# Window attention and two feed-forward layers: the order of GpSimd's early work, and who rounds the second layer's weights

## What is computed

```python
w = np.exp(weight_gen - np.max(weight_gen, axis=-1, keepdims=True))
w = w / (np.sum(w, axis=-1, keepdims=True) + 1e-09)
x_pad = np.concatenate([np.zeros((B, pad, D)), x], axis=1)      # pad = 6
out = np.einsum('bshk,bskhg->bshg', w, x_unf)                   # x_unf: windows of 7 tokens
...
h = x @ moe_w_in;   g = h * np.cos(h);            x = g @ moe_w_out
h = x @ moe2_w_in;  g = np.maximum(0.01 * h, h);  y = g @ moe2_w_out
```

## Time and profile before

| | us |
|---|---|
| median of 3 runs | 1169.44 (1168.51 to 1169.97) |
| the profiled execution | 1169.68 |
| its span, first to last instruction | 1167.8 |
| TensorE busy | 1144.5 (98%) |
| VectorE busy | 898.7 (77%) |
| ScalarE busy | 735.3 (63%) |
| GpSimd busy | 88.1 (8%) |

### The profile page before, as it was taken

One profiled execution on the slowest core, in us unless ns is written; L12 is line 12 of the kernel. 1 busy time (PEld: TensorE's weight loads), 2 busy tenths in 40 slices (PEclk: granted clock), 3 DMA queues, 4 the chain that ended last, 5 costly groups with the idle time before them and its releaser, 6 DMA issues.

```text
span 1167.8 us, 23296 instructions
## 1 busy us (share of the span) xinstructions
PE 1144.5 (98%) x10170; PEld 953.3 (82%) x10170; DVE 898.7 (77%) x860; ACT 735.3 (63%) x804; POOL 88.1 (8%) x89
## 2 busy tenths in 40 slices
PE   7789999999999999999999999999999999999998
PEld 5668888888888888888888888888888888888876
DVE  7778797778978788697786968868697786968433
ACT  5566675666757666575665757566575665757544
POOL 5761000000000000000000000000000000000000
PEclk9989999999999999999999999999999999999999
DMA  9700101001010010101001010010101001000000
GB/s 270 200 2 1 35 1 49 1 1 49 1 49 1 4 45 1 49 1 49 1 1 49 1 49 1 15 35 1 48 2 49 1 1 48 1 15 1 15 1 28
DMA packets 17389, 34.25 MB, mean 29 GB/s; under 512 B 5132, under 2 KB 11658, under 8 KB 17032
## 3 DMA queue, kind: packets, MB, share of 16 engines
q1 hardware_dynamic: 15114, 30.90, 8.4%
q0 software_dynamic: 2080, 1.57, 0.7%
q10 hardware_dynamic: 94, 0.29, 0.1%
HBM read 26.46 MB, written 6.29 MB: 28 GB/s over the span
## 4 chain that ended last, share of the span: by engine, by line
PE 92%; DVE 3%; POOL 2%; ACT 1%; issue 1%; DMA 0%; ACTq 0%; POOLq 0%
PE slot L1052 42%; PE acc_a L1052 28%; PE acc_b L1052 18%; DVE prods L304 1%; DVE g_lo L813 1%; POOL out_hi_lo L542 1%; DVE prods L298 1%; POOL prods L298 1%; POOL prods L304 1%; DMA taps_w<-in_weight_gen 0%; PE slot L997 0%; PE slot L984 0%; POOL in_a_lo L536 0%; DVE gate L885 0%; PE acc_b L1025 0%
## 5 line engine op out<-in xcount | busy, mean ns | idle before, releaser
L1052 PE MATMUL acc_a<-g_hi,out_hi_lo 64*128 64x512 f32 x2000 | 695.9, 388 | 0.0
L1052 PEld LDWEIGHTS acc_a<-g_hi,out_hi_lo 64*128 64x128 f32 x2000 | 368.0, 184 | 35.9
L1052 PE MATMUL acc_b<-g_hi,out_hi_lo 64*128 64x512 f32 x1000 | 387.9, 388 | 0.3 <-DVE g_lo L813 0.3
L1052 PE MATMUL acc_a<-g_lo,out_hi_lo 64*128 64x512 f32 x1000 | 386.5, 387 | 0.0
L1052 PE MATMUL acc_b<-g_lo,out_hi_lo 64*128 64x512 f32 x1000 | 386.4, 386 | 0.0
L813 DVE TENSOR_TENSOR g_lo<-gate,g_hi 128x1024 fp32r<-128x1024 f32 x240 | 293.0, 1221 | 117.2 <-ACT g_hi L624 116.8
L624 ACT ACTIVATE g_hi<-gate 128x1024 fp32r<-128x1024 f32 x240 | 254.4, 1060 | 90.8 <-PE acc_b L1052 77.5
L1052 PE MATMUL slot<-x_a_hi,in_a_lo 64*128 64x512 f32 x1024 | 299.9, 394 | 5.6 <-DVE g_lo L813 3.8
L1052 PE MATMUL slot<-x_b,in_b_hi 64*128 64x512 f32 x1024 | 296.2, 387 | 0.2 <-DVE x_b L827 0.2
L1052 PE MATMUL slot<-x_a_lo,in_a_hi 64*128 64x512 f32 x1024 | 296.2, 387 | 0.0
L1052 PE MATMUL slot<-x_a_hi,in_a_hi 64*128 64x512 f32 x1024 | 296.1, 387 | 0.0
(11 more groups left out here) (99 smaller groups left out, 1095.6 us busy)
## 6 DMA issues: line engine op xcount, KB each, us to landing
x_win<-in_x SPq DMA_DIRECT2D x14, 960.0 KB, 4.7
out<-result SPq DMA_DIRECT2D x16, 384.0 KB, 2.3
out_raw<-in_moe_w_out SPq DMA_DIRECT2D x3, 512.0 KB, 10.4
out_hi_lo<-in_moe_w_out POOLq DMA_DIRECT2D x2, 768.0 KB, 16.3
taps_w<-in_weight_gen SPq DMA_DIRECT2D x2, 560.0 KB, 7.9
in_a_raw<-in_moe_w_in SPq DMA_DIRECT2D x1, 1024.0 KB, 12.2
in_b_raw<-in_moe_w_in SPq DMA_DIRECT2D x2, 512.0 KB, 15.1
out_raw<-in_moe_w_out SPq DMA_DIRECT2D x1, 1024.0 KB, 21.9
```

The source lines that it names most:

```text
L1052: return nc.tensor.matmul(to, w[rows, :], x[rows, :], start=start, stop=stop)
```

## The change

1. `stays` holds for iteration 0 alone; first-layer units of iteration 1 write their results to `gate`.
2. GpSimd no longer waits for the second softmax's subtraction ahead of its column lows. Piece 2 of W1.out's lows goes behind the sum of pairs of chunk 1, piece 3 behind all of chunk 1's attention, with a wait for its end (`att` 22).
3. W2's high parts come by four transfers that round on the way, on GpSimd's queue behind piece 3. GpSimd's copies and casts for W2 go, the differences stay. SP loads `in_b_lo_raw` of W2 in its final layout, and waits for W1.out's second rounding transfer ahead of W2's raw loads. The zero borders of W2's `in_b_hi` are made by subtracting the identity from itself instead of by memsets.
4. The whole first halo is issued on SP. In chunk 0 the second and third product are split: the part that needs own tokens alone comes first, then the rest behind the halo's wait.

```diff
@@ stays @@
-        return i <= 1 and q < len(FIRST_UNITS)
+        return i == 0 and q < len(FIRST_UNITS)
@@ attention @@
+            def product(k, to, j, until):
+
+                w = taps_w[:, (c * J + j) * heads:(c * J + until) * heads, k]
+                return engine.tensor_tensor(
+                    prods[:, to, j * dim:until * dim].rearrange("p (r g) -> p r g", g=group),
+                    view[:, (k + j) * heads:(k + until) * heads, :],
+                    w.unsqueeze(2).to_broadcast([P, (until - j) * heads, group]), ALU.mult)
...
-                tap(4, 2)
+                product(4, 2, 0, J if c else 2).then_inc(att, 1)
 
             def start():
                 wait_for_chunk()
 
                 tap(6, 0)
+                if c == 0:
+                    product(5, 1, 1, J)
+                    product(4, 2, 2, J)
 
             def rest_of_window():
                 wait_for_halo()
-                tap(5, 1)
+                product(5, 1, 0, J if c else 1).then_inc(att, 1)
@@ SP @@
             load_own(0)
+            load_halo(sp, 0, 0)
             load_halo(sp, 0, P // batch)
...
+            sp.wait_ge(out_hi_loaded[1], 16)
             sp.dma_start(W2.in_a_raw[:, :], w_in2[0:DA, :]).then_inc(w2_loaded[0], 16)
-            sp.dma_start(W2.in_b_raw[0:DB, P:], w_in2[DA:dim, :])\
-                .then_inc(w2_loaded[1], 16)
-            sp.dma_start(W2.in_b_raw[DB:P, 0:hidden], w_in2[DA:dim, :])\
-                .then_inc(w2_loaded[1], 16)
+            for t in range(PAIR):
+                sp.dma_start(W2.in_b_lo_raw[t * DB:(t + 1) * DB, :].rearrange("p (u c) -> p u c", c=P),
+                             w_in2[DA:dim, :].rearrange("p (u t c) -> p u t c", t=PAIR, c=P)[:, :, t, :])\
+                    .then_inc(w2_loaded[1], 16)
@@ GpSimd @@
             pool.wait_ge(w1_first_lo, 2)
-            pool.wait_ge(soft, soft_count(1, "subtract"))
...
             for instruction in of_pool[:2]:
                 instruction()
-            for n in range(1, len(OUT_PIECES)):
-                out_lows(n)
-            for instruction in of_pool[2:]:
+            out_lows(1)
+            of_pool[2]()
+            out_lows(2)
+            for instruction in of_pool[3:]:
                 instruction()
+
+            pool.wait_ge(att, 2 * ATT_STEPS)
+            out_lows(3)
+            pool.dma_start(W2.in_a_hi[:, :], w_in2[0:DA, :]).then_inc(w2_hi_loaded[0], 16)
+            pool.dma_start(W2.in_b_hi[0:DB, P:], w_in2[DA:dim, :]).then_inc(w2_hi_loaded[1], 16)
+            pool.dma_start(W2.in_b_hi[DB:P, 0:hidden], w_in2[DA:dim, :]).then_inc(w2_hi_loaded[1], 16)
+            pool.dma_start(W2.out[:, :, 0:dim], w_out2.rearrange("(f p) d -> p f d", p=P))\
+                .then_inc(w2_hi_loaded[2], 16)
 
             pool.wait_ge(lo_ready, unit(0, 6) + 1)
             pool.wait_ge(w2_loaded[0], 16)
-            for n, cols in enumerate(W2_PIECES):
-                pool.tensor_copy(W2.in_a_hi[:, cols], W2.in_a_raw[:, cols])\
-                    .then_inc(w2_hi, 1)
-                pool.wait_ge(w2_hi, n + 1)
+            pool.wait_ge(w2_hi_loaded[0], 16)
+            for cols in W2_PIECES:
                 pool.tensor_tensor(W2.in_a_lo[:, cols], W2.in_a_raw[:, cols],
                                    W2.in_a_hi[:, cols].bitcast(FP32), ALU.subtract).then_inc(w2_lo, 1)
...
@@ ScalarE @@
-            load_halo(act, 0, 0)
             exponentials(0)
```

More of the change, by code:

```diff
@@ L231, in window_attention_two_ffn @@
         out_hi_loaded = [sem(f"out{n}_hi_loaded") for n in range(2)]
+        w2_hi_loaded = [sem(f"w2_{n}_hi_loaded") for n in ("a", "b", "out")]
         padded = sem("padded")
@@ L240, in window_attention_two_ffn @@
         w1_out_lo = sem("w1_out_lo")
-        w2_hi = sem("w2_hi")
         w1_raw = sem("w1_raw")
-        w2_raw = sem("w2_raw")
         w2_lo = sem("w2_lo")
@@ L294, in attention @@
             view = window[:, :, :].rearrange("p t (h g) -> p (t h) g", g=group)
-            def tap(k, to):
-                w = taps_w[:, c * J * heads:(c + 1) * J * heads, k]
-                engine.tensor_tensor(
-                    prods[:, to, :].rearrange("p (r g) -> p r g", g=group),
-                    view[:, k * heads:(k + J) * heads, :],
-                    w.unsqueeze(2).to_broadcast([P, J * heads, group]), ALU.mult).then_inc(att, 1)
+            def product(k, to, j, until):
[4 more added lines that the diff above has]
+                    w.unsqueeze(2).to_broadcast([P, (until - j) * heads, group]), ALU.mult)
+            def tap(k, to):
+                product(k, to, 0, J).then_inc(att, 1)
             def add(to, a, b):
@@ L519, in _ @@
             pool.memset(g_hi[:, 0, :].bitcast(FP32), 1.0).then_inc(clock_ready, 1)
-            for n, w in enumerate((W1, W2)):
-                if n:
-                    pool.wait_ge(padded, 2 * n)
-                pool.memset(w.in_b_raw[0:DB, 0:P], 0.0).then_inc(padded, 1)
-                pool.wait_ge(padded, 2 * n + 1)
-                pool.memset(w.in_b_raw[DB:P, hidden:], 0.0).then_inc(padded, 1)
-            pool.wait_ge(padded, 4)
+            pool.memset(W1.in_b_raw[0:DB, 0:P], 0.0).then_inc(padded, 1)
+            pool.wait_ge(padded, 1)
+            pool.memset(W1.in_b_raw[DB:P, hidden:], 0.0).then_inc(padded, 1)
+            pool.wait_ge(padded, 2)
+            for n, (rows, cols) in enumerate(((slice(0, DB), slice(0, P)),
+                                              (slice(DB, P), slice(hidden, hidden + P)))):
+                pool.tensor_tensor(W2.in_b_hi[rows, cols], ident[rows, :], ident[rows, :], ALU.subtract)\
+                    .then_inc(padded, 1)
+                pool.wait_ge(padded, 3 + n)
             pool.wait_ge(in_loaded[2], 48)
@@ L576, in _ @@
             pool.wait_ge(w2_loaded[1], 32)
-            pool.tensor_copy(b_lows(W2.in_b_lo_raw, every), b_pairs(W2.in_b_raw, every)).then_inc(w2_raw, 1)
-            pool.wait_ge(w2_raw, 1)
-            pool.tensor_copy(W2.in_b_hi[:, :], W2.in_b_raw[:, :]).then_inc(w2_hi, 1)
-            pool.wait_ge(w2_hi, len(W2_PIECES) + 1)
+            pool.wait_ge(w2_hi_loaded[1], 32)
             pool.tensor_tensor(b_lows(W2.in_b_lo, every), b_lows(W2.in_b_lo_raw, every),
@@ L583, in _ @@
             pool.wait_ge(w2_loaded[2], 32)
-            for n, f in enumerate(OUT_PIECES):
-                for high, _, raw in out_parts(W2, f):
-                    pool.tensor_copy(high, raw).then_inc(w2_hi, 1)
-                pool.wait_ge(w2_hi, len(W2_PIECES) + 3 + 2 * n)
+            pool.wait_ge(w2_hi_loaded[2], 16)
+            for f in OUT_PIECES:
                 for high, low, raw in out_parts(W2, f):
```

## The result

The changed kernel takes **1166.25 us** (median of 7 runs, 1164.16 to 1166.69) where the kernel before takes 1169.44 (7 runs beside them, 1168.51 to 1170.94): a ratio of **0.9969 [0.9957, 0.998]**, 3.2 us less. The forecast was 1163.4, in a range of 1161.4 to 1166.6. The sign and the range held; of the forecast 6.0 us about half arrived. The profiled execution took 1166.25 us, its span is 1164.4 against 1167.8.

What follows compares the result with a forecast made beforehand. TensorE, busy 98% of the span, was taken as the bound, so only its idle time could be won. 4.15 + 0.4 + 1.25 - 0.3 + 0.5 = 6.0 us gave a median of 1163.4, range 1161.4 to 1166.6.

Steps and rivals of the forecast that it cites:

- Step 1: GpSimd's new order avoids its wait for W1.out; its last product ends at 52.1 instead of 56.27: 4.15 us won.
- Step 2: TensorE's idle ahead of the second transposes shrinks from 6.2 to 2.6 us, so the clock's fall goes: 0.4 us.
- Rival B: The start wins nothing and the clock falls all the same: 0.9 to 1.4 us less, 1164.3 to 1165; chance 0.11.
- Steps 3 and 4: Iteration 1's PSUM slots free earlier, 1.25 us won; its g_lo meet GpSimd's W2 lows, 0.3 us lost.
- The term of -0.3 for the port: In iteration 1, VectorE's g_lo wait for running GpSimd instructions: 0.3 us lost, bounds 0 and 3 us.
- Rival A: Three to five g_lo of iteration 1 wait up to 1.3 us each at the port: 1165 to 1166.5; chance 0.15.
- Step 5: At the start, earlier weights outweigh the cost of splitting VectorE's first products: net 0.5 us won, bounds -0.5 and +1.0.
- Step 6: W2's four rounding transfers land before TensorE wants them near 101: cost 0, with 15 us of cover.
- the step's own bound from below: At the pace of stores, W2's 3.5 MB of rounding transfers take 21 us, landed by 80.
- Rival D: W2 comes late, at W1.out's transfer pace, and the kernel is slower: 1171 to 1189; chance 0.04.

Runs made afterwards that it cites:

- both_back: The changed kernel with GpSimd's old order restored and SP's wait ahead of W2's raw loads removed; 1166.15 us, ratio 0.9970 to the kernel before.
- after_again: The changed kernel itself, unaltered, measured and profiled once more; 1166.63 us, ratio 0.9969 to the kernel before.
- start_back: The changed kernel with half of the first halo back on ScalarE's queue and chunk 0's products unsplit; 1167.21 us, ratio 0.9975 to the kernel before.
- slots_back: The changed kernel with iteration 1's first units writing results into the PSUM slots again; 1166.14 us, ratio 0.9968 to the kernel before.

## Why the prediction was right, and where it was not

**Step 1, GpSimd's order: the size right, the credit wrong.** Forecast: sum of pairs at 38.3, last product's end 52.1, transposes 56.4 and with the start's 0.5 us 55.9. Measured: 38.01, 51.73, 56.04. The first product took 1.18 us instead of 2.15, as the reading of the earlier trace rows wanted. But the wait of 4.20 us would have gone without the new order: both_back keeps the old one and waits 0.53 us. The step listed W2's loads as what stands beside W1.out's transfer, credited SP's hold, and never asked what the smaller loads do by themselves. The change removes the wait in more ways than one, so that the number came out does not speak for the step's reason.

**Step 2, the clock: the step that failed.** "So I take the fall as gone." The 0.4 us up to the pair came (0.43: 6.11 us from transposes to pair before, 5.68 now). The fall did not go, it moved: from 57.4 to 64.3, where TensorE stood or had slack behind it, to 62.5 to 65.9, where it had no idle time. There the matmuls took 0.62 us instead of 0.39, and 1.6 us were lost. The step looked at one gap by itself. Two gaps were left, 1.16 and 2.48 us, with the transposes and ten products between them. The second had been 1.30 before: the step took that wait as a sign that the ten products cost nothing, and did not ask what the gap behind them becomes when they run at the full clock. By after_again the loss is not in every execution. In the profiled one it is over half of the missing 2.3 us at the second fold. Rival B held the fall, but at 0.4 us, the price of the harmless place.

**Steps 3 and 4, the slots and the port: right in kind, 0.95 forecast, some 0.5 measured.** The wait of 1.67 us became one of 1.23 within the unit, where 0.4 were forecast, since g_lo took 1.93 us. The term of -0.3 for the port should have been -0.7; 0.7 lies within its bounds of 0 to 3. Rival A, three to five long g_lo in a row, did not happen in the change (the third took 1.23 us), but after_again came near it: 1.64, 1.38 and 1.93 us, 1.3 us more than three of 1.21. The Trainium skill (SBUF — State Buffer, "SBUF: two separate sides") says that a VectorE instruction with two SBUF inputs and a GpSimd instruction that reads SBUF contend for one port pair, which is an exclusive lock for the whole instruction. The traces agree: the first product and the multiply at 24.47 ended 0.81 and 0.48 us behind the end of the GpSimd instruction that they met, and take 0.95 and 0.62 us alone. The small operation at 4.53 has a single input and met a memset, which is not that case; it ended 0.17 us behind the memset and takes 0.18 alone.

**Step 5, the start: 0.5 forecast, 0.84 by start_back.** The weights landed 2.2 us earlier (5.05 to 2.84), not 0.9. Of that, 1.0 us went at the memset (1.18 against 0.18) and 0.2 in the split products (3.79 against 3.56), which the step had put at 0.4 to 0.5. What reached the splits of the first transposes, 0.86 us (20.78 against 21.64), was lost to the multiply at 24.47 by part 2 of the change: step 1 had priced the meeting of GpSimd's lows and the second softmax at 0.62 us for GpSimd and at nothing for VectorE.

**Step 6, W2's transfers: right.** TensorE had no wait near 95 us. W2.out, the last, let GpSimd go on at 71.99, 16.3 us behind the first issue at 55.71; the step's own bound from below gave 21 us. The estimate from the Trainium skill (DMA: Bandwidth & Descriptors, "Anatomy of one DMA — SWDGE (gpsimd) path") was some 16 us. Rival D is out.

**What no step had.** From the second fold to the end the change lost 0.3 us against the execution before, after_again 1.0 and slots_back 1.25. Some 0.35 us of it go between two folds: from the eleventh to the twelfth the kernel before took 34.68 us (430.20 to 464.88), the change 35.02 (426.44 to 461.46). All twelve profiles with the split products of part 4 show 35.02 to 35.12 there, and start_back, which undoes part 4, took 34.67. So it goes with part 4; no run shows why. The rest of the loss in after_again and slots_back is spread evenly over the span, and its cause is open too.

## What to carry to other kernels

When a long gap is made shorter, the clock's fall may come later, in the dense work behind it, where it costs in full. Look at each gap that is left, and at what it becomes when the work ahead of it runs at the full clock. If one can't be closed, it can be filled with products nobody reads, which must end before the wait is over. A single profile can miss this: look at the granted clock of every execution. Where a wait for a transfer goes with a change, look at what travels beside the transfer before crediting the order of instructions. Between VectorE and GpSimd on SBUF, less than 0.1 us in who comes first was worth 1 us, so an instruction moved a little earlier may come out later.

## What was not expected of the hardware

- The place of the clock's fall differs between executions of one kernel (62.5 to 65.9 and 57.9 to 61.3), and with it 1.6 us.
- The first 112 KB landed 2.84 us into the span, 2.1 us behind their issue, when ScalarE's queue sent nothing; before, 4.3. start_back, with ScalarE's halo back, had them at 4.98.
- A memset, which reads nothing, held up VectorE's small operation with a scalar: 1.18 us instead of 0.18. GpSimd can be held up in turn: 3.76 us for two products instead of 3.05, and 9.83 us for eight lows instead of 7.81.
- Halving 1 MB of loads beside a rounding transfer, in shorter rows, let that transfer land about 5 us earlier (40.5 to 35.5), if the elimination holds.
- Splitting two products at the start went with 0.35 us more between two folds far behind it, at 426 and 461 us.
